# Bucket-masked attention and two MLPs: heads laid out transposed by the host, plain float32 for bits and values, and a new order of work

## The reference, cut to what matters

```python
# q, k, v: (2, 8, 768, 64), proj: (64, 6)
q_bits = einsum('bhsd,dk->bhsk', q, proj) > 0      # k_bits likewise
mask = q_bucket[:, :, :, None] == k_bucket[:, :, None, :]
scores = where(mask, q @ k.T / sqrt(64), -1e9)
attn = softmax(scores);  x = attn @ v              # x becomes (1536, 512)
h = x @ w_in0                                      # (1536, 2048)
g = (a0 + a1*h + a2*h**2 + a3*h**3) / (1 + |b0|*|h| + |b1|*h**2)
x = g @ w_out0                                     # (1536, 512)
h = x @ w_in1;  out = (h * clip(h + 3, 0, 6) / 6) @ w_out1
```

## Time and the profile before

| | |
|---|---|
| median of 3 runs | 817.36 us (817.24 to 818.34) |
| profiled execution, its own time | 818.54 us |
| span of that execution | 816.8 us |
| granted TensorE clock, mean | 0.998 |
| busy: PE, DVE, ACT, POOL | 96%, 67%, 61%, 35% of the span |
| chain that ended last, by engine | PE 75%, DVE 8%, issue 7%, ACT 6%, POOL 2%, DMA 1% |

### The profile page before, as it was taken

One profiled execution on the slowest core, in us unless ns is written; L12 is line 12 of the kernel. 1 busy time (PEld: TensorE's weight loads), 2 busy tenths in 40 slices (PEclk: granted clock), 3 DMA queues, 4 the chain that ended last, 5 costly groups with the idle time before them and its releaser, 6 DMA issues.

```text
span 816.8 us, 13110 instructions
## 1 busy us (share of the span) xinstructions
PE 787.6 (96%) x3968; PEld 665.4 (81%) x3968; DVE 548.8 (67%) x929; ACT 501.4 (61%) x950; POOL 283.8 (35%) x457
## 2 busy tenths in 40 slices
PE   4999999999999889999999999999999999999998
PEld 4898888988888668888888888888888888888886
DVE  3899899989998678888988898893222322232223
ACT  2788887888889789877676688984222122212221
POOL 2887777877777844410000024442000000000000
PEclk9999999999999999999999999999999999999999
DMA  5221221222111233310000013331000100010001
GB/s 153 61 63 52 79 60 50 61 79 60 50 42 48 72 84 103 94 37 0 0 0 0 1 48 97 98 95 51 1 1 0 52 0 0 0 45 7 0 1 52
DMA packets 33568, 36.67 MB, mean 45 GB/s; under 512 B 3136, under 2 KB 25664, under 8 KB 33536
## 3 DMA queue, kind: packets, MB, share of 16 engines
q1 hardware_dynamic: 33536, 36.26, 15.7%
HBM read 26.22 MB, written 3.15 MB: 36 GB/s over the span
## 4 chain that ended last, share of the span: by engine, by line
PE 75%; DVE 8%; issue 7%; ACT 6%; POOL 2%; DMA 1%; ACTq 0%; DVEq 0%; SPq 0%; POOLq 0%
PE y_ps L954 32%; PE h_ps L888 10%; PE h_ps L889 10%; PE h_ps L887 10%; PE o_ps L866 4%; PE t_ps L854 3%; PE s_ps L844 2%; ACT probs L450 2%; ACT pt_hi L459 2%; DVE pt_lo L655 2%; PE s_ps L845 2%; DVE neg_max L641 2%; PE p_ps L817 1%; DVE q_main L635 1%; DVE o_pair L664 1%
## 5 line engine op out<-in xcount | busy, mean ns | idle before, releaser
L728 DVE SCALAR_TENSOR_TENSOR t_abs<-t_abs,h_ps 128x512 f32<-128x512 f32 x48 | 33.0, 688 | 187.1 <-ACT t_abs L525 187.1
L399 POOL TENSOR_TENSOR slot<-w_raw,slot 128x512 fp32r<-128x512 f32 x64 | 81.5, 1293 | 206.2 <-ACT slot L478 206.2
L525 ACT ACTIVATE t_abs<-h_ps,three_col 128x512 f32<-128x512 f32 x48 | 33.1, 689 | 191.1 <-PE h_ps L889 191.0
L887 PE MATMUL h_ps<-x_hi,slot 128*128 (+1 forms) x384 | 150.1, 391 | 0.2 <-DVE t_num L709 0.2
L889 PE MATMUL h_ps<-x_hi,slot 128*128 (+1 forms) x384 | 150.2, 391 | 0.0
L888 PE MATMUL h_ps<-x_lo,slot 128*128 (+1 forms) x384 | 150.0, 391 | 0.0
L954 PE MATMUL y_ps<-g_hi,slot 128*128 128x512 f32 x384 | 126.2, 390 | 0.4 <-DVE g_lo L734 0.4
L954 PE MATMUL y_ps<-slot,g_hi 128*128 128x512 f32 x384 | 118.3, 389 | 0.0
L450 ACT ACTIVATE probs<-s_ps,exp_bias,exp_scale 128x768 f32<-128x768 f32 x96 | 95.5, 995 | 35.4 <-POOL exp_bias L386 34.7
L655 DVE TENSOR_TENSOR pt_lo<-t_ps,pt_hi 128x384 fp32r<-128x384 f32 x192 | 97.3, 548 | 17.9 <-ACT pt_hi L459 16.8
L641 DVE TENSOR_REDUCE neg_max<-s_ps 128x1 f32<-128x768 f32 x96 | 91.5, 953 | 11.3 <-PE s_ps L845 10.0
(11 more groups left out here) (102 smaller groups left out, 1416.6 us busy)
## 6 DMA issues: line engine op xcount, KB each, us to landing
w_raw<-in_moe_w_in SPq DMA_DIRECT2D x32, 256.0 KB, 2.7
w_raw<-in_moe_w_out SPq DMA_DIRECT2D x32, 256.0 KB, 2.7
raw_qk<-in_q SPq DMA_DIRECT2D x16, 192.0 KB, 2.4
raw_qk<-in_k SPq DMA_DIRECT2D x16, 192.0 KB, 2.5
raw_v<-in_v SPq DMA_DIRECT2D x16, 192.0 KB, 2.4
q_main<-q_cross SPq DMA_DIRECT2D x16, 192.0 KB
k_main<-k_cross SPq DMA_DIRECT2D x16, 192.0 KB
out<-t_den SPq DMA_DIRECT2D x6, 256.0 KB, 2.1
```

The costliest lines, as they stand in the source:

```text
L399: nc.gpsimd.tensor_tensor(slots[f][:, j, 1, :], w_raw[j][:, :], slots[f][:, j, 0, :].bitcast(F32), ALU.subtract).then_inc(w_lo_made, 1)
L887: mm(h_ps[b][:, :], w_hi, x_hi[:, kt, cols], start=(kt == 0), stop=False)
```

## The change

- **Host.** q and k come to the kernel transposed, (b, h, d, n), with the order of rows that the kernel's tiles use. GpSimd's splitting before the transposes, the transposes on TensorE and ScalarE's copies of them go. A raw tile [128, 768] has q on rows 0 to 63 and k on rows 64 to 127. ScalarE rounds it whole to q_main (split_hi), GpSimd subtracts it whole to q_cross (split_lo), and SyncE moves the pieces that belong elsewhere.
- **Bits** are plain-float32 matmuls with 32 stationary columns, on four column quarters of the array: two heads times two halves of 384 columns, once a pair. One comparison per pair writes a tile bits, and four moves of 12 rows x 384 columns per head bring them into q_main and k_main.
- **Values.** The turned probabilities are kept once, in float32: ScalarE copies one half, VectorE the other. Each value matmul is plain float32, 64 stationary columns, 384 moving; the two heads of a pair write the two halves of rows of one bank. A group of 12 goes in three runs of four, at steps 1, 3 and 5 of a head, one pair late. No v split, no cross, no addition. x_hi and x_lo are made per group straight from the bank.
- **Bias.** The second small operation of GpSimd reads the first one's result and waits for it. The scale of the scores goes in there.
- **Weights.** Five slots are split from pair 2 on, one a pair, instead of six in the last pair and the drain.
- **Drain.** A new order, written out below. The loops over pairs are unrolled in the program.

```diff
 # SyncE
+            def place_head(h):
+                u = h % 2
+                sp.wait_ge(hi_made, h + 1)
+                move(k_main[u][0:D, :], q_main[u][D:P, :]).then_inc(moved_in[u], 16)
+                move(k_cross[u][0:D, :], q_main[u][D:P, :]).then_inc(moved_in[u], 16)
+                if h > 0:
+                    sp.wait_ge(lo_made, h + 1)
+                    move(k_cross[u][D:P, :], q_cross[u][D:P, :]).then_inc(moved_in[u], 16)
+                    sp.wait_ge(moved_in[u], 48 * (h // 2 + 1) - (16 if u == 0 else 0))
+                move(q_cross[u][D:P, :], q_main[u][0:D, :]).then_inc(main_in[u], 16)
+                if h == 0:
+                    sp.wait_ge(moved_in[u], 32)
+            def place_bits(h):
+                i, u = divmod(h, 2)
+                sp.wait_ge(bits_made, i + 2 if h else 1)
+                for half in range(2):
+                    cols = slice(HALF * half, HALF * (half + 1))
+                    at = QUAD * (2 * u + half)
+                    move(q_main[u][D:KROWS, cols], bits[at:at + MASKROWS, :]).then_inc(main_in[u], 16)
+                    move(k_main[u][D:KROWS, cols], bits[at + MASKROWS:at + 2 * MASKROWS, :]).then_inc(main_in[u], 16)
...
+            for h in range(NHEAD):
+                i, u = divmod(h, 2)
+                if h + 1 < NHEAD:
+                    place_head(h + 1)
+                if u == 0 and i >= 1:
+                    load_v(i)
+                if u == 0 and EARLY_PAIR <= i < EARLY_PAIR + EARLY_SLOTS:
+                    load_weights(0, i - EARLY_PAIR)
+                if h + 1 < NHEAD:
+                    place_bits(h + 1)
+                if h >= 1 and h + 3 < NHEAD:
+                    sp.wait_ge(lo_made, h)
+                    sp.wait_ge(bits_dot, (h - 1) // 2 + 2)
+                    load_raw((h + 3) // 2, (h + 3) % 2)
 # GpSimd
+            def split_lo(h):
+                u = h % 2
+                alone(hi_made, h + 1)
+                nc.gpsimd.tensor_tensor(q_cross[u][:, :], raw[h // 2 % 2][u][:, :], q_main[u][:, :].bitcast(F32),
+                                        ALU.subtract).then_inc(lo_made, 1)
...
                     bias(n, j)
-                    if within(n - 1, NTILE):
+                    if n >= 1:
                         normalise(n - 1, j - 1)
...
+                    if j % TILES == 1 and h + 1 < NHEAD:
+                        split_lo(h + 1)
 # ScalarE, a step
+                if t == 0 and 3 <= h < NHEAD - 1:
+                    upper_x(h - 3)
+                if n >= 1:
                     exponentials(n - 1, j - 1)
+                if t == 0 and h + 1 < NHEAD:
+                    split_hi(h + 1)
+                if n >= TURN_LAG:
+                    take_turned(n - TURN_LAG)
 # ScalarE, the drain
+            exponentials(NTILE - 1, NTILE - 1)
+            act.wait_ge(exped, NTILE)
+            read_h(0, 0, 0)
+            take_turned(NTILE - 3)
+            take_turned(NTILE - 2)
+            seed(0, 0)
+            upper_x(2 * PAIRS - 2)
+            take_turned(NTILE - 1)
...
 # VectorE, a step
+                maximum(n, j)
+                if n >= 1:
                     invert(n - 1, j - 1)
...
+                if t == 0 and 3 <= h < NHEAD - 1:
+                    lower_x(h - 3)
+                if n >= TURN_LAG:
+                    take_turned(n - TURN_LAG)
+                if j == PROJECT_AT + 1 and i + 1 < PAIRS:
+                    threshold(i + 1)
 # VectorE, the drain
+            denominator(0, 0)
+            numerator(0, 0)
+            take_turned(NTILE - 3)
+            take_turned(NTILE - 2)
+            divide(0, 0)
+            lower_x(2 * PAIRS - 2)
+            take_turned(NTILE - 1)
...
 # TensorE
+                for half in range(2):
+                    at = QUAD * (2 * u + half)
+                    last = mm(p_ps[at:at + QUAD, 0:HALF], proj_pair[:, :],
+                              raw[i % 2][u][:, HALF * half:HALF * (half + 1)], start=True, stop=True)
...
+                for kt in some:
+                    for u in range(2):
+                        last = mm(weigh_bank(e)[D * u:D * (u + 1), 0:HALF], v_nat[i % 2][u][:, kt, :],
+                                  pt(i, u, g)[:, kt, :], start=(kt == 0), stop=(kt == TILES - 1))
...
+                scores(h, i, u, n, j, t)
+                if n >= TURN_LAG:
+                    for half in range(2):
+                        turn_probs(n - TURN_LAG, half)
+                if i == PAIRS - 1 and j in LAST_WEIGH:
+                    weigh(i - 1, *LAST_WEIGH[j])
+                if 1 <= i < PAIRS - 1 and t in WEIGH_AT:
+                    weigh(i - 1, u, WEIGH_AT[t])
+                if j == PROJECT_AT and i + 1 < PAIRS:
+                    project(i + 1, 0)
+                    project(i + 1, 1)
...
+            hidden(0, 0, 0, 0)
+            for n in (NTILE - 3, NTILE - 2):
+                for half in range(2):
+                    turn_probs(n, half)
+            weigh(PAIRS - 1, 0, tuple(range(TILES)))
+            for half in range(2):
+                turn_probs(NTILE - 1, half)
+            hidden(1, 0, 0, 1)
+            weigh(PAIRS - 1, 1, tuple(range(TILES)))
```

More of the change, by code:

```diff
@@ L510, in _ @@
-            with act.Fori(1, PAIRS - 1) as i:
-                for j in range(2 * TILES):
-                    step(i, j)
             def read_h(m, n, b):
@@ L572, in _ @@
                     tile(0, f, f % 2)
-                else:
-                    seed(1, 1)
                 if f - 1 + EARLY_SLOTS < FT:
@@ new lines, in _, with threshold @@
+            nc.vector.tensor_tensor(k_cross[0][D:P, :], raw[0][0][D:P, :], q_main[0][D:P, :].bitcast(F32),
+                                    ALU.subtract).then_inc(lo_made, 1)
+            def threshold(i, rows=slice(0, P), first=False):
+                dve.wait_ge(bits_dot, 1 if first else i + 2)
+                if i >= 1:
+                    dve.wait_ge(main_in[1], 80 * i)
+                nc.vector.tensor_scalar(bits[rows, :], p_ps[rows, 0:HALF], bit_col[rows, 0:1], bit_col[rows, 1:2],
@@ L695, in _ @@
+            dve.wait_ge(bit_col_in, 32)
+            threshold(0, slice(0, D), first=True)
+            threshold(0, slice(D, P))
+            for i in range(PAIRS):
                 for j in range(2 * TILES):
@@ L801, in _ @@
             mm = nc.tensor.matmul
-            def turn_natural(h, u, part, bank):
-                src = (nat_q, nat_k)[part // 2][u]
-                if isinstance(h, int) and h == 0:
-                    pe.wait_ge(first_split, 2 * (part // 2) + 2)
-                    after(pe, qk_copied, part - 1)
-                elif part:
-                    pe.wait_ge(qk_step, 4 * h + 2 * (part // 2) + 2)
-                    pe.wait_ge(qk_copied, 4 * h + part)
-                else:
-                    pe.wait_ge(qk_step, 4 * h + 2)
-                    pe.wait_ge(bits_made, 2 * h)
-                half = part % 2
-                for s in range(GROUP):
-                    last = nc.tensor.transpose(bank[:, P * s:P * (s + 1)].bitcast(F32R),
-                                               src[:, GROUP * half + s, :, :].rearrange("p a d -> p (a d)"),
-                                               ident_r[:, :])
-                last.then_inc(qk_turned, 1)
@@ L903, in step @@
                 h, n = 2 * i + u, 2 * TILES * i + j
-                early, late = ((0, 1), (2, 3), (None, 4), (None, 5), (None, None), (None, None))[t]
-                ahead = within(h + 1, NHEAD)
-                if within(n, NTILE):
-                    scores(h, i, u, n, j, t)
-                if ahead and early is not None:
-                    prepare(h + 1, 1 - u, early)
-                if within(n - TURN_LAG, NTILE):
-                    for half in range(2):
-                        turn_probs(n - TURN_LAG, j - TURN_LAG, half)
@@ L914, in step @@
-                gj, third = divmod(j - WEIGH_LAG, GROUP)
-                if within(4 * i + gj, NGROUP):
-                    weigh(4 * i + gj, 2 * i + gj // 2, gj, third)
-                if ahead and late is not None:
-                    prepare(h + 1, 1 - u, late)
-            pe.wait_ge(dve_setup, 1)
-            pe.wait_ge(sel_made, 9)
-            for part in range(6):
-                prepare(0, 0, part)
-            for j in range(2 * TILES):
-                step(0, j)
-            with pe.Fori(1, PAIRS - 1) as i:
+                scores(h, i, u, n, j, t)
```

513 lines of the change are left out of this document (192 added, 321 removed).

## The result

| | before | changed |
|---|---|---|
| median of the runs compared | 817.79 us (817.24 to 818.34, 5 runs) | 825.55 us (822.16 to 826.37, 5 runs) |
| span of the profiled execution | 816.8 us | 822.5 us |
| granted TensorE clock, mean | 0.998 | 0.979 |

The ratio is 1.0088 (95% interval 1.0075 to 1.0101): 0.9% slower. The profiled execution of the changed kernel took 824.72 us, 2.2 more than its span.

The account below looks back on a forecast made before the run. Bound: the chain of moves through SyncE's queue at head changes. Start 14.5, head changes 246.2, clock 4.2, drain 34 and MLP 521.7 sum to a span of 820.6; prediction 821 us, range 796 to 844.

Parts of the forecast that it names:

- the mechanism named first: Attention head changes: hand-offs through SyncE's queue end last and stall TensorE 1.5 to 3 us a head; chance 0.45.
- first score: Start of the kernel: more small loads and later bit moves put it at 14.5 us instead of 13.72.
- seven odd heads: Attention heads without value or weight loads in SyncE's queue: 15.8 us each, 110.6 in sum.
- seven even heads, weight loads in five: Attention heads with two value loads queued: 16.5 us each, 0.75 more in five with weight loads.
- the clock: Even heads: after stalls the clock halves, t0's scores take 1.3 instead of 0.71, seven times 0.6: 4.2 us.
- drain: From the last head's first score to the gapless MLP part: 34 us against 35.0 before, gain 1.
- The chain through SyncE: Each head change: subtraction, k move, its landing, q move, four bit moves at 0.79; last lands 15.8 after first score.
- S: Time of a head's first score, from which the prediction counted the steps to the next head.
- B: Faster rival: bit moves issue at 0.34 to 0.50 us, deciding below 0.70; 800 to 804 us; chance 0.13.
- The price e: Time of one plain-float32 matmul of 384 columns on TensorE: taken as 0.3 us, bounds 0.17 and 0.83.
- A: Slower rival: plain-float32 matmuls on two column halves don't overlap, about 0.65 us each; 840 us; chance 0.27.
- C: Fastest rival: the hand-off chain doesn't bind, tile ring with split_lo sets 14.4 us a head; 787 us; chance 0.10.

Follow-up runs that it names:

- experiment 2: Changed kernel with value loads queued behind the bit moves on SyncE and early weight loads issued one head earlier: 803.23 us, 0.9823 of the kernel before.
- experiment 3: Changed kernel with the 128x768 lower-half subtraction moved from GpSimd to VectorE, at step t = 1 of a head: 802.22 us, 0.9810 of the kernel before.
- Experiment 5: Changed kernel with only the early weight loads issued one head sooner, value loads still ahead of the bit moves: 814.52 us, 0.9954 of the kernel before.
- kernel 8: Changed kernel with 16-row bit moves, value loads later, weight loads earlier, subtraction on VectorE, turned tiles first in the drain: 785.26 us, 0.9596 of the kernel before.
- experiment 4: Changed kernel with the same value matmuls ordered all of one head, then all of the other: 841.67 us, 1.0284 of the kernel before.
- experiment 6: Changed kernel with eight extra, unused plain-float32 matmuls of 128 columns at the end of each head: 830.56 us, 1.0139 of the kernel before.
- Experiment 7: Changed kernel with ScalarE and VectorE taking two turned tiles before reading the first hidden tile in the drain: 820.58 us, 1.0023 of the kernel before.
- experiment 10: kernel 8 with the value matmuls of one head after those of the other: 826.42 us, 1.0092 of the kernel before.
- experiment 1: Changed kernel with each of the four bit moves taking 16 rows instead of 12: 820.41 us, 1.0043 of the kernel before.

## Why the prediction was right, point by point

821.0 was predicted, 825.55 measured. Slower was right, and the mechanism named first is what the even heads show. In the odd heads it was not what ended last, and that their sum came out exactly is luck.

| term | predicted | measured |
|---|---|---|
| first score | 14.5 | 15.28 |
| head 0 | 16.3 | 15.16 |
| seven odd heads | 110.6 | 110.6 |
| seven even heads, weight loads in five | 119.3 | 122.8 |
| the clock | 4.2 | in the three rows above |
| drain | 34 | 38.10 |
| MLP part | 521.7 | 520.6 |
| span | 820.6 | 822.5 |

Of the 4.6 us that the time is over, 1.9 are in the span. They are what is left of larger misses both ways: the start, the even heads and the drain are 8.4 over, head 0, the clock's own term and the MLP part 6.4 under. The other 2.6 come from turning the span into a time. I added 0.4, having set the median before (817.36) against the span of an execution that took 818.54, 1.7 more than its span; here the execution took 2.2 more than its span, and the median stands another 0.8 above it.

**The chain through SyncE.** In the even heads right, step by step. In head 10, a head with weight loads, the k move was issued at S + 7.4 (predicted 8.05), the q move 2.5 after it (2.4), the bit moves from S + 12.6 on take 0.80, 0.78, 0.72 and 0.71 (0.79 each), the next scores start 2.0 after the last of these issues starts (2.4), and the head takes 16.98 (17.25). The price of 12 rows, read from the one such move of before, was the step that decided between this case and B; the median is 0.749, above B's turning point of 0.70. Experiments 2, 3 and 5 each shortened another link or took loads out of it, and each took 10 us or more off the head changes.

**Odd heads.** The prediction had them at 15.8 by the same chain, with TensorE ready at S + 14.2 and a stall of 1.5 to 3 us. They took 14.86 to 17.02, and but for head 1 they ended without a stall. TensorE's own work is longer than I had it: the bits' matmuls (0.79) lie in these heads, so that it takes 14.9, as in heads 3 and 11 of this kernel (14.86, 15.01) and in the odd heads of kernel 8 from head 3 on; and in heads 5, 7, 9 and 13 the slow clock adds 0.9 to 2.1. In experiment 3 the chain of head 3 ends earlier, its last bit move issued 3.56 us before the next scores and not 2.04, and the head still takes 14.85. The chain was not far off, though: in the changed kernel the last moves of these heads landed less than 1 us before the scores. That 110.6 comes out of both accounts is luck. The even heads' stalls cost the odd heads too, by way of the clock.

**The price e.** Predicted 0.3, measured 0.36, against the bounds 0.17 and 0.83. What the prediction took from the skill on four passes and on tiles side by side is borne out. Alone a matmul takes 0.68 (experiment 4), four times the 0.17 of the earlier trace rows, as "FP8 and Floating Point Precision" of the Trainium skill, TensorE Precision Notes, has it. In pairs it takes about half, which "TensorEngine Tiling (Array Packing)", Key Properties, leads one to expect. That page's drain at a change of mode is small here: the run of four takes 1.44 us, its inner spacing is 0.32, so at most 0.16 is left for both ends.

**Even heads.** Predicted at 17.25 with weight loads, the five took 17.8. I had the weight loads as two issues (0.75) only. Not foreseen was ScalarE in front of the weights with an exponential behind it. I had named what is queued behind SyncE's wait, but not who waits for the loads queued there. Experiment 5 shows that this costs more than the issues. In heads 6 and 8 the profile names ScalarE's exponential, and not a move, as the last that the next scores waited for.

**The clock.** It does fall inside the attention part, after stalls of even heads, as predicted. Busy time by stretch, from one head's first score to the next, heads 3 and 5 to 8 of 0 to 15, and one matmul of head 7:

```profile
63.87:78.73 14.86, 14.42 (x93) 9.35 (x93) 9.94 (x20) 8.94 (x19) 9.24 (x19) 1.00 0.35 85
...
96.29:112.09 15.80, 15.80 (x92) 10.82 (x93) 10.25 (x22) 10.75 (x22) 12.37 (x21) 0.89 0.34 81
112.09:129.27 17.18, 13.96 (x86) 9.24 (x85) 9.23 (x20) 10.45 (x22) 10.04 (x20) 1.00 0.47 127
129.27:145.34 16.07, 16.03 (x93) 10.45 (x93) 10.44 (x22) 10.62 (x22) 12.35 (x21) 0.89 0.37 90
145.34:164.40 19.06, 13.97 (x87) 9.24 (x85) 9.25 (x20) 10.47 (x22) 10.08 (x20) 0.93 0.42 109
...
130.91 0.67 PE L776 MATMUL s_ps<-k_cross,q_cross 128*128 128x512 f32 x1
```

The stall stands at the end of an even head (TensorE busy 13.96 of 17.18 us), and the slow matmuls are those of the odd head behind it (0.89). I had t0's scores slow. In head 7 they start at 129.27 with 0.47, at full clock; t1's are the first slow ones (0.67). The heads themselves give a price: an odd head at full clock takes 14.86 to 15.01, at 0.87 to 0.89 it takes 15.80 to 16.16, and in the kernel of experiment 3 it is 14.85 to 14.91 against 15.78 and 15.81. By an estimate from these rows, heads 5, 7, 9 and 13 lost 5.4 us to the slow clock, against the 4.2 of my term. No run takes the clock away by itself: experiment 6 lengthened what it was to cover. In kernel 8, where TensorE hardly stalls, the mean is 0.999.

**The drain.** The term furthest off, by 4.1 us. TensorE in order of time:

```profile
280.64 0.50 PE L823 MATMUL h_ps<-x_hi,slot 128*128 128x512 f32 x1 [1.52 <-DVE x_lo L617]
...
286.14 0.52 PE L786 MATMUL t_ps<-ident,probs 128*128 128x128 f32 x3 [1.83 <-ACT pt_second L443]
288.39 0.87 PE L786 MATMUL t_ps<-ident,probs 128*128 128x128 f32 x3 [1.73 <-DVE pt_second L611]
289.20 0.90 PE L803 MATMUL o_ps<-pt_first,v_nat 128*64 128x384 f32 x1
```

hidden(0) starts 16.8 after the last head's first score, where I had 14.5, and behind two waits for the copies of turned tiles the weighing, 0.49 to 0.54 a record elsewhere, starts at 0.90. Experiment 7 takes the reads of the hidden tile out of the way of both copies and gives 3.3 of it back.

**The start.** 0.8 late: the last bit move is issued at 13.19, not at 12.0, since the value loads came at 9.82 and the landing took 2.1.

**The rivals.** A fell with e = 0.36; experiments 4 and 10 show that it would have come true with another order of the same matmuls. B's condition doesn't hold (0.749), and its mechanism is shown in part only: at 0.59 an issue its own count gives 15 x 3 x 0.16 = 7.2 from the head changes, where experiment 1 has 1.4. Its 800 should have been 797 by its own numbers, 821 less 20 for the moves and 4 for the clock. C had the chain ending before TensorE's own work in every head; that occurred in the odd heads from head 3 on, and not in the even ones. The rate it named, 14.4 us a head, is what kernel 8 reaches (14.5), with the chain shortened by hand.

## What to carry to other kernels

When work is taken off busy engines and given to a DMA queue as hand-offs, follow one unit of work through that queue, with every issue, wait and landing, and compare the sum with the unit's period: here 12 rows by 384 columns cost 0.75 us to issue, and four of them in a row, behind a wait and behind loads, let every second head start 1.3 to 4.9 us late, whatever the engines had less to do. Look at the matmuls' own idle time before calling a wait a stall: a wait of the weight load alone cost nothing here. A stall can also be paid twice, by the wait and by the slow clock behind it. Put loads that nobody needs soon behind the moves that the next head needs, and ask for each load behind a wait which engine sits in front of it and what is queued behind that engine. When edits to such a chain are tried singly their gains don't add: stop when the next bound (here 14.5 us a head) is reached.

## What the runs showed of the hardware

- Two streams of plain-float32 matmuls on different column halves overlap almost fully: 0.36 us for one of 384 columns, 0.68 when neighbours use the same half. With a mixed order at the border of the two heads in experiment 4, records of both heads still start together (144.61 and 144.62). Four column quarters: the bits' eight records start at 170.69 and the next scores at 171.48, 0.20 us for each of the four matmuls.
- An in-SBUF move of 384 columns takes 0.749 us to issue with 12 rows and 0.590 with 16; one of 64 rows and 768 columns takes 0.46 to 0.60.
- Where the matmuls stood idle for the bit moves, the scores start 2.00 us after the start of the last move's issue (before heads 3 and 11).
- The 128x768 subtraction takes 0.96 us on VectorE and 1.83 on GpSimd, not the 2 x 1.005 that half-size operations on GpSimd gave before.
